# Who splits the first two heads' q and k: GpSimd in the first rounds, or ScalarE and VectorE

## The reference

```python
scores = scale * np.matmul(q, k.transpose(0, 1, 3, 2))        # batch 4, 8 heads, 576 positions, head size 64
rel = (pos[:, None] - pos[None, :]).astype(np.float32)
psi_rel = np.log1p(np.abs(rel))
psi_i = np.log1p(np.maximum(pos[:, None].astype(np.float32), 1.0))
x = (psi_rel / psi_i)[..., None]
h = np.maximum(x @ w1 + b1, 0.0)                              # 32 hidden values for each pair of positions
bias = h @ w2                                                 # one value for each head
scores = scores + bias.transpose(2, 0, 1)[None, :, :, :]
...
attn = attn / (np.sum(attn, axis=-1, keepdims=True) + 1e-09)
return np.matmul(attn, v).astype(np.float32)
...
x = _moe_ref(x=x, **moe_kwargs)
return _moe2_ref(x=x, **moe2_kwargs)
```

## Time and profile before

| | |
|---|---|
| median of 3 runs | 1204.89 us (1204.81 to 1205.14) |
| the profiled execution | 1205.83 us, its span 1204.0 us |
| TensorE busy | 1168.5 us, 97% |
| VectorE busy | 672.8 us, 56% |
| ScalarE busy | 495.7 us, 41% |
| GpSimd busy | 489.3 us, 41% |
| mean granted TensorE clock | 0.997 |

### The profile page before, as it was taken

The page is one execution under the profiler, slowest core; times in us unless marked ns, Lnnn a source line. Parts: engine busy times, 40 slices in busy tenths (PEclk is TensorE's granted clock), DMA queues, the critical chain, the costliest instruction groups (busy, mean ns, idle before and its releaser), DMA issues. The chain is left out here.

```text
span 1204.0 us, 21829 instructions
## 1 busy us (share of the span) xinstructions
PE 1168.5 (97%) x7464; PEld 1077.1 (89%) x7464; DVE 672.8 (56%) x1540; ACT 495.7 (41%) x1034; POOL 489.3 (41%) x515
## 2 busy tenths in 40 slices
PE   5789999999989999999999999999999999999998
PEld 2257777777779999999999999999999999999998
DVE  8978888888879856667575786553021020210201
ACT  6977787777723433433343333111121111211211
POOL 3057777777766342524242362751111111111111
PEclk9999999999999999999999999999999999999999
DMA  5854435352144000000000010330000000000000
GB/s 181 242 182 125 162 101 168 100 188 87 50 114 123 18 2 1 0 0 0 0 0 0 0 41 29 106 114 27 1 1 26 0 26 0 0 26 0 26 0 26
DMA packets 46535, 69.06 MB, mean 57 GB/s; under 512 B 3713, under 2 KB 27425, under 8 KB 46497
## 3 DMA queue, kind: packets, MB, share of 16 engines
q1 hardware_dynamic: 46496, 68.60, 18.3%
HBM read 53.25 MB, written 15.34 MB: 57 GB/s over the span
## 5 line engine op out<-in xcount | busy, mean ns | idle before, releaser
L818 PE MATMUL banks<-x_high,w_high_rest 128*128 128x384 f32 x672 | 225.3, 335 | 0.0
L820 PE MATMUL banks<-x_high,w_low_rest 128*128 128x384 f32 x672 | 224.6, 334 | 0.0
L819 PE MATMUL banks<-x_low,w_high_rest 128*128 128x384 f32 x672 | 224.5, 334 | 0.0
L1388 POOL TENSOR_TENSOR product_low<-X,product_high 128x384 fp32r<-128x384 f32 x72 | 72.9, 1013 | 346.0 <-ACT product_high L1331 346.0
L1369 DVE TENSOR_TENSOR X<-X,banks 128x384 f32<-128x384 f32 x72 | 39.8, 552 | 298.4 <-PE banks L820 298.4
L1186 POOL TENSOR_TENSOR product_low<-g,product_high 128x384 fp32r<-128x384 f32 x96 | 103.6, 1079 | 234.6 <-ACT product_high L1068 234.1
L818 PE MATMUL bank<-product_high,w_high_rest 128*128 128x384 f32 x480 | 161.2, 336 | 0.0
L820 PE MATMUL bank<-product_high,w_low_rest 128*128 128x384 f32 x480 | 160.4, 334 | 0.0
L819 PE MATMUL bank<-product_low,w_high_rest 128*128 128x384 f32 x480 | 160.4, 334 | 0.0
L644 DVE CUSTOM_DVE_ANT_0 probs<-banks,bias 128x576 f32<-128x576 f32 (+1 forms) x160 | 119.5, 748 | 18.8 <-PE banks L506 9.2
L594 ACT ACTIVATE probs<-probs,neg_max 128x576 f32<-128x576 f32 (+1 forms) x160 | 123.3, 771 | 8.6 <-DVE neg_max L644 7.3
(11 more groups left out here) (113 smaller groups left out, 2540.5 us busy)
## 6 DMA issues: line engine op xcount, KB each, us to landing
raw_qk<-in_qk SPq DMA_DIRECT2D x32, 576.0 KB, 3.7
bias_scratch<-bias_stage SPq DMA_DIRECT2D x36, 288.0 KB, 3.1
bias<-bias_scratch SPq DMA_DIRECT2D x32, 288.0 KB, 3.6
w_raw<-in_w_out SPq DMA_DIRECT2D x28, 256.0 KB, 2.6
values<-in_v SPq DMA_DIRECT2D x16, 320.0 KB, 4.0
w_raw<-in_w_in SPq DMA_DIRECT2D x16, 256.0 KB, 2.9
out_t<-X SPq DMA_DIRECT2D x5, 768.0 KB, 3.5
w_raw<-in_w_gate SPq DMA_DIRECT2D x12, 256.0 KB, 3.1
```

The source lines that it names most:

```text
L818: nc.tensor.matmul(out, high, x_high, start=start, stop=False)
L819: nc.tensor.matmul(out, high, x_low, start=False, stop=False)
L820: return nc.tensor.matmul(out, low, x_high, start=False, stop=stop)
L1388: pool.tensor_tensor(sl[f % 2][:, :], s, sh[f % 2][:, :].bitcast(F32), ALU.subtract).then_inc(s_split, 1)
```

## The change

The high parts of the first pair's q and k are made by ScalarE, as four copies behind its round 0, and not by GpSimd. The low parts are made by VectorE: three behind its last round of the bias stage, the fourth (q of head 1) as its first operation of attention. GpSimd has no q or k in the bias stage any more. Since `raw_qk` is now free only when VectorE has made the low parts, SyncE's loads of pair 1's q and k move behind the barrier: head 0's between bias tiles 4 and 5, head 1's behind tile 9.

```diff
@@ SyncE, bias stage @@
             with sp.Fori(0, EARLY // 4) as m:
                 store(m)
-            for h in range(2):
-                att.load_qk(sp, 1, h, False)
@@ GpSimd, bias stage @@
             att.setup(pool)
-            att.prepare(pool, 0, 0)
-            att.prepare(pool, 0, 1)
@@ ScalarE, bias stage @@
             groups(0, 0, 0)
+            for h in range(2):
+                att.first_high_parts(act, h)
             act.wait_ge(shift_ready, 2)
@@ VectorE, bias stage @@
                 groups(m * 2 + 1, 1, 2)
+            att.low_part_k(dve, 0, 0)
+            att.low_part_q(dve, 0, 0)
+            att.low_part_k(dve, 0, 1)
@@ class Attention @@
-    def prepare(self, pool, n, h):
-        self.high_part(pool, n, h, False, True)
-        self.high_part(pool, n, h, True, True)
-        self.low_part_k(pool, n, h)
-        pool.wait_ge(self.k_low_ready, n * 2 + h + 1)
-        self.low_part_q(pool, n, h)
+    def first_high_parts(self, act, h):
+
+        act.wait_ge(self.qk_in[h], 16)
+        act.activation(self.q_parts[h][:, 0:S], self.raw_q[h], ACT.Copy).then_inc(self.high_ready, 1)
+        act.activation(self.k_high[h][:, :], self.raw_k[h], ACT.Copy).then_inc(self.high_ready, 1)
@@ SyncE, attention @@
-            for s in range(EARLY_TILES, TILES):
-                att.load_bias(sp, 0, s, True, 0)
+            for h in range(2):
+                for s in range(max(h * NQ, EARLY_TILES), (h + 1) * NQ):
+                    att.load_bias(sp, 0, s, True, 0)
+                att.load_qk(sp, 1, h, False)
@@ VectorE, attention @@
+            att.low_part_q(dve, 0, 1)
             pair(0, 0, 0, hp=0)
```

## The result

| | before | changed |
|---|---|---|
| median, 22 runs each | 1204.93 us | 1203.02 us |
| range | 1204.3 to 1206.32 | 1201.75 to 1204.93 |
| profiled execution, its span | 1205.83, 1204.0 | 1201.75, 1200.0 |

The ratio is 0.9984, 95% interval 0.9978 to 0.9990: 1.9 us faster, between 1.2 and 2.7. In two later comparisons the same kernel gave 0.9986 (0.9977 to 0.9995; 11 runs) and 0.9979 (0.9970 to 0.9988; 11 runs). The forecast was 3.3 us. So the sign and the range held, and the size was too large by 1.4 us; the gain of over 0.2% that it held likely came out at 0.16%.

A forecast was written before the change was run, and what follows sets the result against it. VectorE bounds the bias stage, VectorE and through it GpSimd the border, TensorE whole stretches from about 88 us. Gain 4.4 less loss 1.1 gives −3.3 us: median 1204.89 to 1201.6, range 1200.2 to 1203.9.

The forecast's parts named there:

- The slow round is GpSimd's doing: Bias stage: VectorE's round from 10.58 lasts 9.12 us instead of 4.42 because GpSimd's eight q and k operations run beside it.
- Gain 4.4 us: Bias stage: without GpSimd's eight operations VectorE's round 3 starts at 19.7 instead of 24.12; bounds 3.7 to 4.9 us.
- TensorE's third block of round 0 ... ends at 12.7 whatever VectorE does: Bias stage: this block starts at 11.60, ends at 12.7; VectorE's last four operations of round 1 wait for it, 12.8 to 14.8.
- ScalarE's four copies: ScalarE's idle time 8.04 to 10.70: four 128x576 copies at a pace of 0.6 us, so its round 1 starts at 10.8.
- copies hold ScalarE up: Part of a rival, chance 0.07: copies of 1.7 us each delay ScalarE's rounds and TensorE, gain gone, 1204.9 to 1206.
- VectorE's four subtractions at no cost: Bias stage's end and attention's start: three hidden by the barrier's wait for SyncE, one by VectorE's wait for TensorE; cost 0.
- Loss 1.1 us: Border: head 0's load between tiles 4 and 5 makes VectorE wait 1.1 us for tile 5; bounds 0 to 2.8.
- Both paths are late by the same 1.1: Border: VectorE's wait for tile 5 and GpSimd's chain from pair 1's q each lose 1.1 us, not the sum.
- The clock: Rival, chance 0.05: waiting for tile 5 lowers TensorE's clock again just after; +0.6 us, 1202.2.
- the border costs more: Rival, chance 0.12: pair 1's load takes as long as the slower measured pair of transfers; loss 2.8, gain 4.4, 1203.3.
- The border is free: Rival, chance 0.14: the moved transfer slips between tiles with slack, only the gain of 4.4 us is left, 1200.5.
- Slower: Rival, chance 0.05: GpSimd's chain bounds the border; slower than before if pair 1's q lands after 78.6; 1206.4 at 9.8 after issue.

The follow-up runs named there:

- both heads loaded early: Changed kernel, pair 1's q and k of both heads loaded at the old early place into unused parts of X: 1200.78 us, later 1201.11 us.
- head 0 loaded early: Changed kernel, only head 0's q and k of pair 1 loaded at the old early place into an unused part of X: 1201.26 us (5 runs).
- changed, 24 products: Changed kernel plus 24 unneeded TensorE products behind the bias stage's last block, to shorten TensorE's pause before attention: 1203.06 us (10 runs).
- both loads behind tile 9: Changed kernel, with both heads' q and k of pair 1 loaded behind bias tile 9: 1207.76 us (10 runs), 1.0017 of before.
- both early, 8 products: Changed kernel with pair 1's q and k loaded early for both heads, plus eight unneeded TensorE products behind the bias stage: 1201.27 us (6 runs).
- low parts by GpSimd: Kernel before, with only the four high parts moved to ScalarE; GpSimd keeps the low parts, pair 1's loads stay early: 1204.41 us against 1205.07.
- GpSimd busy again: Changed kernel with eight unneeded GpSimd operations of the old sizes put back beside the first rounds: 1207.04 us against 1203.70 for the changed kernel.

## Why the prediction was right, and where it was not

- **The slow round is GpSimd's doing**: right, and settled by putting the work back.
- **Gain 4.4 us**: the first profile gives 4.44 at TensorE's first score, the second 4.1, the third 3.4 (against 67.61, the mean of before): 4.0 in the mean. The step that is off is "TensorE's third block of round 0 ... ends at 12.7 whatever VectorE does". It ends at another time in each execution. In the third profile VectorE waits 1.82 us for it:

```profile
11.98 2.15 PE L254 MATMUL bias_ps<-hidden_last,w2blk 128*32 128x288 f32 x16
...
14.31 2.05 DVE L221 TENSOR_SCALAR hidden_last<-log_table,slope,neg_b 128x576 f32<-128x576 f32 x4 [1.82 <-PE bias_ps L254]
```

  In the kernel before no such wait exists, because the slow round covered it. I had taken one execution's 12.7 for a constant. The bound of 3.7 for the gain came from other causes and was not low enough for the third profile.

  What moves the block is TensorE's clock at the program's start, which no term of the prediction has. The trace's records of the granted clock begin with the full level, at 10.5 to 14.2 us; for the time ahead of the first record the views print 1.00, but the products there take what they take at 0.50. In the nine executions with this bias stage:

| profile | first clock record | the block of 16 products | VectorE's round 3 |
|---|---|---|---|
| changed | 10.5 | 1.14 | 19.60 |
| both heads loaded early | 11.3 | 1.14 | 19.86 |
| changed, second | 12.0 | 1.26 | 19.90 |
| head 0 loaded early | 13.1 | 1.73 | 20.19 |
| changed, 24 products | 13.3 | 1.82 | 20.30 |
| both loads behind tile 9 | 13.5 | 1.98 | 20.35 |
| both early, 8 products | 13.7 | 1.99 | 20.56 |
| both heads loaded early, second | 14.1 | 2.15 | 20.68 |
| changed, third | 14.2 | 2.15 | 20.69 |

  The later the clock rises, the later round 3 starts, without an exception, and the block is never shorter. Against the kernel before (24.12 and 24.07, its first records at 11.2 and 13.2) the gain is 3.4 to 4.5, in the mean 3.9. The second profile of before has the same kind of block at a granted clock of 0.52 (20 to 21 us) and 0.50 after it, and there it takes 1.94:

```profile
19.78 1.94 PE L253 MATMUL bias_ps<-hidden_last,w2blk 128*32 128x288 f32 x16 [0.78 <-DVE hidden_last L223]
```

  So ahead of the first record TensorE ran at the lower of its two levels, 1.2 GHz. It had been at work since about 8.1 us. No run changes the clock there alone; this is read from the order of nine executions, not from an experiment.
- **ScalarE's four copies**: 0.67 each at a pace of 0.58 (forecast 0.69 and 0.6), round 1 at 10.44, 10.75 and 10.84 in the three profiles (forecast 10.8). Right. Nothing came of "copies hold ScalarE up".
- **VectorE's four subtractions at no cost**: right. 0.75 each; the three end at 61.66, the barrier waits for SyncE (its drain at 62.6); the fourth runs 63.02 to 63.78 and VectorE then still waits 0.91 for TensorE.
- **Loss 1.1 us**: too small; by the medians on one chip 1.8. By the profiles it is 1.7: pair 1 comes 13.1 us after the first load in the mean of the five with a load of q and k ahead of tile 5, and 11.3 in the mean of the six whose pair 1 is loaded early for both heads (before twice, low parts by GpSimd, both heads loaded early twice, and with 8 products). The mechanism is right: VectorE waits for tile 5. Two things are missing.
  - The start was one execution. Tile 5 landed 5.0 us after SyncE's first issue there (69.29, the line below, to 74.3). In all eight profiles without a load ahead of it, it took 5.0 to 6.8, 5.5 in the mean; in the five with it, 6.6 to 7.6, 7.2 in the mean. So 576 KB in that place, with their issue, cost 1.7 us in the mean, near the 1.4 (1.6 with the issue) that I took from the quiet pair of the earlier trace rows and far from the busier pair's 3.2. VectorE's use of tile 5, counted from the same issue, is 1.2 later in the mean (the six against the five), about the forecast 1.1. A single execution shows anything from 0.96 to 2.09 as the wait.

```profile
69.29 3.55 SPq L323 DMA_DIRECT2D bias<-bias_scratch  x7
```

  - **"Both paths are late by the same 1.1"** is the step that is off. From VectorE's use of tile 5 to TensorE's pair 1 it is 5.27 to 5.40 us in the six profiles with both loads early and 5.83 to 5.86 in the five with the late one, 0.5 more each time. GpSimd's k_low, begun late behind q, now lies wholly beside VectorE's normalisation behind the next tile, which takes 1.23 to 1.43 us in those five and 0.50 to 1.00 in the six. It looks like the slow round's mechanism again; no run takes it apart.
- **The page's price**: the Trainium skill (SBUF — State Buffer, "A bandwidth-pool intuition that's wrong (but worth ruling out)") has about 358 GB/s from HBM to a core. The 1.65 us, an estimate from it for these bytes, and the row's 1.4 lie on either side of what the profiles show in the mean, 1.5 when the issue's 0.2 is taken off the 1.7. The spread of single executions can't tell the two apart.
- **The clock**: it did fall longer, 61.7 to 68.5 us against 69.3 to 72.7, and the first two tiles' scores are 0.24 us apart instead of 0.13, so VectorE starts 1.49 after TensorE and not 0.93. The rival took the wait for tile 5 as the cause. The fall came before that: in the pause at the barrier in the first two profiles, 1.2 us behind it in the third, and no second fall follows the wait in any of the three. (In the kernel with GpSimd busy again one does, at 82.5 us, 6 us behind the wait.) The cost of this fall does not show in the time; what the clock costs at the program's start does.
- **The sum**: with the measured terms, a gain of 3.9 and a loss of 1.7 to 1.8, it is 2.1 to 2.2 us, and the three comparisons gave 1.9, 1.8 and 2.6. That the forecast was off by 1.4 is the gain taken 0.5 too high and the loss 0.6 to 0.7 too low, both to the same side.
- **Rivals**: "the border costs more" (1203.3) came nearest to the median, but by two terms that cancel: its loss, 2.8, was 1 us too high and its gain, 4.4, 0.5 too high. "The border is free" was the kernel with the early loads (forecast 1200.5, measured 1200.8 and 1201.1), so its arithmetic held for another kernel than the changed one. "Slower" was shown by the loads behind tile 9.

## What to carry to other kernels

Work on GpSimd that nothing waits for is not free where VectorE bounds the stage: here 9.9 us of it cost VectorE 5.4. When such work is moved, look for what had to move with it: the loads that reuse its buffer went from a place where they cost nothing into the one list of loads that the next stage waits for, and took 1.8 of 4.4 us back; a spare buffer gave that back. And a wait that a slow stretch has hidden (TensorE's first round here) is no constant, nor is the arrival of a load: read both in more than one execution before they become terms of a sum.

## What the runs showed of the hardware

- Single operations of VectorE (128x576, float32, SBUF to SBUF) last 0.57 us alone, 0.92 beside GpSimd's copies and 1.28 to 1.68 beside its subtractions; copies of ScalarE at 8 to 10 us left no mark on them (five in 2.54, four in 2.04).
- TensorE's clock rises from the lower to the upper level between 10.5 and 14.2 us, another time in each of 13 executions of kernels that give TensorE the same work up to there. The same 16 small products took 1.14 to 2.15 us for it, and the bias stage's gain varied by 1.1 us.
- The mean granted clock of a run goes with its time. The kernel before took 1204.6 us at 0.999 (mean of 6 runs) and 1205.9 at 0.995 (12 runs); the changed kernel 1202.7 at 0.999 (5 runs) and 1204.4 at 0.995 (7 runs).
- TensorE's clock falls at a border in one execution and not in the next of the same kernel. TensorE's timeline of the kernel before, first profile, at the border behind attention (start us, duration us):

```profile
335.91 0.69 PE L818 MATMUL banks<-x_high,w_high_head 128*128 128x384 f32 x1
...
337.16 3.01 PE L546 MATMUL bank<-probs_t,values 128*64 128x288 f32 x16
```

  The granted clock is 0.50 there. In the changed kernel's first profile the last of them takes 2.16 at full clock. From pair 1's first score to the end the kernel before needed 1123.9 us and the changed kernel 1122.6, so 1.3 of the 4.0 us between the two first profiles arise behind everything that the change touches. The other eleven profiles, none with a fall there, have 1122.3 to 1123.2. So about 1 us of it is the clock's, and some tenths differ without a fall.
